# Attention, then a two-layer feed-forward: 16 leftover groups of v summed for four units at once, and the rests of the features moved to GpSimd

## The reference

```python
q_d, k_d, v_d = (t.reshape(B, H, S // 4, 4, D).mean(axis=3) for t in (q, k, v))
out_up = np.repeat(softmax_attention(q_d, k_d, v_d), 4, axis=2)   # pooled: 144 queries, 144 keys
scores = scale * q @ k.T, only where abs(i - j) < 4               # band: 7 keys for each query
out_local = softmax(scores) @ v
x = (out_up + out_local) as (B * S, H * D) = 2304 tokens x 512
h = x @ moe_w_in;  x = (h * sigmoid(h)) @ moe_w_out               # 512 -> 2048 -> 512
h = x @ moe2_w_in; y = (h * sigmoid(1.702 * h)) @ moe2_w_out
```

## Time and profile before

| | |
|---|---|
| median of 3 runs | 808.96 us (808.95 to 809.37) |
| the profiled execution | 808.21 us, span 806.4 us |
| PE busy | 790.0 us (98%) |
| DVE, ACT, POOL busy | 646.0, 530.8, 208.8 us |

### The profile page before, as it was taken

How to read it: one execution, slowest core, us unless ns; L and a number is a source line. 1 busy time by engine, 2 the same in 40 slices (tenths; PEclk the granted TensorE clock), 3 DMA queues, 4 the chain that set the end, 5 groups by cost and what they waited for, 6 DMA issues and landing times.

```text
span 806.4 us, 15771 instructions
## 1 busy us (share of the span) xinstructions
PE 790.0 (98%) x5864; PEld 763.4 (95%) x5864; DVE 646.0 (80%) x905; ACT 530.8 (66%) x849; POOL 208.8 (26%) x203
## 2 busy tenths in 40 slices
PE   9888799999999999999999999999999999999998
PEld 5666599999999999999999999999999999999998
DVE  7999899999898778998678898899555688456466
ACT  5878865677655678555687556678455786465673
POOL 5899977520274220445200000000000000000000
PEclk9999999999999999999999999999999999999999
DMA  8877647787878887677877778868887877878773
GB/s 282 266 249 238 197 150 259 262 298 233 283 236 268 260 315 245 217 261 258 289 267 249 239 250 262 256 224 272 306 275 257 273 249 266 304 250 271 264 256 136
DMA packets 100763, 205.51 MB, mean 255 GB/s; under 512 B 8784, under 2 KB 56400, under 8 KB 100688
## 3 DMA queue, kind: packets, MB, share of 16 engines
q1 hardware_dynamic: 100688, 204.51, 76.0%
HBM read 160.96 MB, written 43.52 MB: 254 GB/s over the span
## 4 chain that ended last, share of the span: by engine, by line
PE 88%; POOL 8%; issue 3%; DVE 1%; ACT 0%; POOLq 0%; DVEq 0%
PE hid L351 43%; PE yp L377 42%; POOL vpair L1038 2%; POOL vavg L1042 1%; PE yp L393 1%; POOL pband L1032 1%; POOL G L1062 1%; POOL G L1063 1%; POOL G L1068 1%; POOL G L1066 1%; POOL x L284 0%; DVE wh L315 0%; PE sc L1342 0%; PE hp L1342 0%; PE pt L1229 0%
## 5 line engine op out<-in xcount | busy, mean ns | idle before, releaser
L351 PE MATMUL hid<-xs,wh 128*128 128x384 f32 x2016 | 351.3, 334 | 0.7 <-issue 0.4
L351 PEld LDWEIGHTS hid<-xs,wh 128*128 128x128 f32 x2016 | 349.3, 188 | 1.7 <-issue 1.4
L377 PE MATMUL yp<-gr,wh 128*128 128x384 f32 x1968 | 342.1, 334 | 0.0
L377 PEld LDWEIGHTS yp<-gr,wh 128*128 128x128 f32 x1968 | 341.2, 188 | 0.1
L306 ACT ACTIVATE wh<-wr 128x1024 fp32r<-128x1024 f32 (+1 forms) x164 | 164.6, 1004 | 149.8 <-PE hid L351 120.0
L569 DVE TENSOR_TENSOR gr<-G,gr 128x768 fp32r<-128x768 f32 x144 | 137.9, 964 | 52.7 <-ACT gr L449 52.7
L449 ACT ACTIVATE gr<-G 128x768 fp32r<-128x768 f32 x144 | 121.8, 845 | 66.9 <-PE yp L377 66.8
L315 DVE TENSOR_TENSOR wh<-wr,wh 128x1024 fp32r<-128x1024 f32 x76 | 95.1, 1251 | 19.0 <-ACT wh L306 18.8
L412 ACT ACTIVATE G<-G 128x1152 f32<-128x1152 f32 x48 | 55.7, 1161 | 0.8 <-DVE G L564 0.8
L533 DVE TENSOR_TENSOR hv<-p,hid 128x384 f32<-128x384 f32 x48 | 26.3, 548 | 29.8 <-PE hid L351 28.0
L559 DVE TENSOR_TENSOR G<-hv,hid 128x384 f32<-128x384 f32 x48 | 26.3, 549 | 28.2 <-PE hid L351 28.2
(11 more groups left out here) (101 smaller groups left out, 748.0 us busy)
## 6 DMA issues: line engine op xcount, KB each, us to landing
wh<-rests SPq DMA_DIRECT2D x72, 512.0 KB, 3.7
wr<-sums_out SPq DMA_DIRECT2D x48, 512.0 KB, 4.7
wr<-in_w_out SPq DMA_DIRECT2D x36, 512.0 KB, 5.2
rests<-wh SPq DMA_DIRECT2D x36, 512.0 KB, 3.5
wr<-sums_in SPq DMA_DIRECT2D x40, 384.0 KB, 4.0
wr<-in_w_in SPq DMA_DIRECT2D x40, 256.0 KB, 3.5
qk<-in_qkT SPq DMA_DIRECT2D x11, 576.0 KB, 4.8
G<-in_w_in SPq DMA_DIRECT2D x12, 512.0 KB, 5.3
```

The lines of the kernel that those rows point to most:

```text
L351: last = eng.matmul(hid[:, at, 0:HALF], lhsT=wh[:, w % SLOTS, part, a % 4, cc * P:(cc + 1) * P], rhs=xs[:, rest, q, cc, :], start=start an ...
L377: last = eng.matmul(yp[:, at + m, 0:HALF], lhsT=wh[:, w % SLOTS, part, p % 4, m * P:(m + 1) * P], rhs=gr[:, p, rest, :], start=start and p ...
```

## The change

The last groups are now 32 instead of 16: a unit's own tile `vn` holds its first 112 groups, in one slot, and the 32 last ones of four units fill one tile of 128 partitions (`vn_last`), which is summed once for four units, into `vlast`. That is done in units 0, 2, 4 and 7, ahead of that unit's own sum. The transposed probabilities and the pooled product are cut at 112 keys instead of at 128, in as many matmuls as before. `vn` needs no zeros, so its two memsets go. The rests of B11, B21, T1, T3 and T2 leave DVE: GpSimd makes those of B11 and B21 whole, in units 5 and 6, and those of T1, T3 and T2 in two halves each, in units 10 to 15. DVE's rests of B22 and T4 at the end now wait for them.

```diff
+        def rest_x(eng, n, q, chunk=None):
             eng.wait_ge(self.x_hi, 7 * n + FILLS.index(q) + 1)
-            eng.tensor_tensor(xs[:, 1, q], features(n, q), xs[:, 0, q].bitcast(F32),
-                              ALU.subtract).then_inc(self.x_lo, 1)
+            at = slice(0, 2) if chunk is None else slice(chunk, chunk + 1)
+            eng.tensor_tensor(xs[:, 1, q, at], features(n, q)[:, at], xs[:, 0, q, at].bitcast(F32),
+                              ALU.subtract).then_inc(self.x_lo if chunk != 0 else self.x_part, 1)
+            if chunk:
+                eng.wait_ge(self.x_part, FILLS.index(q) - 1)
...
-    RESTS = {4: B11, 6: B21, 10: T1, 12: T3, 14: T2}
+    RESTS = {5: (B11, None), 6: (B21, None), 10: (T1, 0), 11: (T1, 1), 12: (T3, 0), 13: (T3, 1), 14: (T2, 0),
+             15: (T2, 1)}
+    LAST_SUMS = {0: 0, 2: 1, 4: 2, 7: 3}
+    LAST_LOADS = {1: 0, 3: 2, 5: 4}
...
+        def summed(n):
+            return n + 1 + sum(i <= n for i in LAST_SUMS)
+        def pooled(u, j):
+            at = u.n % 4 * REST
+            return (slice(0, MOST), slice(0, MOST)) if j == 0 else (slice(MOST, SD), slice(at, at + REST))
...  SyncE
+                    if u.n in LAST_LOADS:
+                        eng.wait_ge(v_sum, summed(LAST_LOADS[u.n]))
+                        load_last(LAST_SUMS[LAST_LOADS[u.n]] + 1)
...  GpSimd, behind pband
+                if u.n in LAST_SUMS:
+                    at = LAST_SUMS[u.n]
+                    eng.wait_ge(last_in, DMA_INC * (at + 1))
+                    sum_groups(vn_last[:], vpair[:], vlast[:, at, :], summed(u.n) - 2)
+                eng.wait_ge(vn_in[u.odd], DMA_INC * (u.half + 1))
                 if u.n > 1:
                     eng.wait_ge(avg_out, u.n - 1)
+                sum_groups(vn[u.odd][0:MOST], vpair[0:MOST], vavg[u.odd][0:MOST], summed(u.n) - 1)
+                if u.n in RESTS:
+                    ffn.rest_x(eng, 0, *RESTS[u.n])
...
+            def sum_groups(groups, pair, to, done):
+                if done:
+                    eng.wait_ge(v_sum, done)
+                eng.tensor_tensor(pair, groups[:, 0:4 * D], groups[:, 4 * D:8 * D], ALU.add).then_inc(v_half, 1)
+                eng.wait_ge(v_half, done + 1)
+                eng.tensor_tensor(to, pair[:, 0:2 * D], pair[:, 2 * D:4 * D], ALU.add).then_inc(v_sum, 1)
...  VectorE
-                elif n in RESTS:
-                    ffn.rest_x(eng, 0, RESTS[n])
                 elif n == UNITS:
                     ffn.rest_weights(eng, 1)
+                    eng.wait_ge(ffn.x_lo, 5)
                     ffn.rest_x(eng, 0, B22)
                     ffn.rest_x(eng, 0, T4)
...
-            for v_rest in vn:
-                eng.memset(v_rest[:, 1, :], 0.0).then_inc(pads, 1)
...  TensorE, avg_product
-                eng.wait_ge(v_sum, u.n + 1)
+                eng.wait_ge(v_sum, summed(u.n))
```

More of the change, by code:

```diff
@@ L100, in __init__ @@
         self.x_half, self.x_sum, self.x_hi, self.x_lo = (sem(n) for n in ("x_half", "x_sum", "x_hi", "x_lo"))
+        self.x_part = sem("x_part")
         self.product, self.pair = sem("product"), sem("pair")
@@ L266, in round_x @@
             eng.activation(xs[:, 0, q], features(n, q), ACT.Copy).then_inc(self.x_hi, 1)
-        def rest_x(eng, n, q):
+        def rest_x(eng, n, q, chunk=None):
             eng.wait_ge(self.x_hi, 7 * n + FILLS.index(q) + 1)
-            eng.tensor_tensor(xs[:, 1, q], features(n, q), xs[:, 0, q].bitcast(F32),
-                              ALU.subtract).then_inc(self.x_lo, 1)
+            at = slice(0, 2) if chunk is None else slice(chunk, chunk + 1)
[3 more added lines that the diff above has]
+                eng.wait_ge(self.x_part, FILLS.index(q) - 1)
         def sum_x(eng, n, q, chunk=None):
@@ L779, in programs, with build @@
         self.round_weights, self.rest_weights = round_weights, rest_weights
-def build(nc, qkT, v, vw, w_in, w_out, out, heads):
+def build(nc, qkT, v, vw, vl, w_in, w_out, out, heads):
     B, H, S, D = heads
@@ L823, in build @@
     SC = 512 - HALF * WIN
-    REST = SD - P
+    REST = P // 4
+    MOST = SD - REST
     NA = 3
@@ L872, in build @@
             VN = FACTOR * 2 * D
[L873 to L877, removed]
+            vlast = sb("vlast", [P, UNITS // 4, 2 * D])
+            vavg = [sb(f"vavg{i}", [P, 2 * D]) for i in range(2)]
+            vn = [sb(f"vn{i}", [P, VN]) for i in range(2)]
+            vn_last = sb("vn_last", [P, VN])
+            vpair = sb("vpair", [P, 2 * D * 2])
             sums4 = sb("sums4", [P, 2, SD])
@@ L914, in build @@
         vn_in = [sem(f"vn_in{i}") for i in range(2)]
+        last_in = sem("last_in")
         qk_in = [sem(f"qk_in{i}") for i in range(3)]
@@ L947, in load_vn, with load_last @@
             def load_vn(u):
[L948 to L952, removed]
+                eng.dma_start(vn[u.odd][0:MOST], v[bass.ds(u.n, 1), :, :].rearrange("a p n -> (a p) n")).then_inc(
+                    vn_in[u.odd], DMA_INC)
+            def load_last(i):
+                eng.dma_start(vn_last[:], vl[bass.ds(i, 1), :, :].rearrange("a p n -> (a p) n")).then_inc(
+                    last_in, DMA_INC)
             def load_vwin(u):
@@ L963, in start @@
                 load_vn(u)
+                load_last(0)
                 load_qk(u.after().after())
@@ L1033, in body @@
                                   ALU.mult).then_inc(b_nrm, 1)
[L1034 to L1039, removed]
+                if u.n in LAST_SUMS:
[3 more added lines that the diff above has]
+                eng.wait_ge(vn_in[u.odd], DMA_INC * (u.half + 1))
                 if u.n > 1:
                     eng.wait_ge(avg_out, u.n - 1)
-                eng.tensor_tensor(vavg[u.odd][:], vpair[:, 0], vpair[:, 1], ALU.add).then_inc(v_sum, 1)
+                sum_groups(vn[u.odd][0:MOST], vpair[0:MOST], vavg[u.odd][0:MOST], summed(u.n) - 1)
+                if u.n in RESTS:
+                    ffn.rest_x(eng, 0, *RESTS[u.n])
                 if not first:
@@ L1068, in sum_weights @@
                     eng.tensor_tensor(at(S4), at(A12), at(S2), ALU.subtract).then_inc(ffn.w0_sum, 1)
-            eng.wait_ge(pads, 5)
+            eng.wait_ge(pads, 3)
             iterations(eng, lambda u: None, body)
@@ L1084, in group @@
                 else:
-                    eng.activation(pta[:, j - NLG, :], src[:, 0:NA * AR], ACT.Copy).then_inc(p_cp, 1)
+                    rows = pooled(u, j - NLG)[1]
+                    eng.activation(pta[rows, j - NLG, :], src[rows, 0:NA * AR], ACT.Copy).then_inc(p_cp, 1)
             def body(u, first, last):
@@ L1100, in body @@
                 if last is None:
-                    eng.wait_ge(v_sum, UNITS)
+                    eng.wait_ge(v_sum, summed(UNITS - 1))
                     ffn.scalar(eng, True)
@@ L1281, in group @@
                 else:
+                    keys, rows = pooled(u, j - NLG)
                     for c in range(NA):
-                        keys = (j - NLG) * REST
-                        last = transpose(to[:, c * AR:(c + 1) * AR], pavg[u.odd][:, c, keys:keys + P])
+                        last = transpose(to[0:rows.stop, c * AR:(c + 1) * AR],
+                                         pavg[u.odd][:, c, keys.start - rows.start:keys.stop])
                 last.then_inc(p_tr, 1)
@@ L1305, in avg_product @@
                 eng.wait_ge(p_cp, 3 + NG * (u.n + 1))
-                eng.wait_ge(v_sum, u.n + 1)
+                eng.wait_ge(v_sum, summed(u.n))
                 for h in range(2):
-                    for j in range(2):
-                        last = eng.matmul(po[h * D:(h + 1) * D, OA:OA + SD], lhsT=vavg[u.odd][:, j, h * D:(h + 1) * D],
-                                          rhs=pta[:, j, :].rearrange("p (c q) -> p c q", c=NA)[:, :, h * QT:h * QT + AQ],
+                    for j, pool in enumerate((vavg[u.odd], vlast[:, u.n // 4, :])):
+                        rows = pooled(u, j)[1]
+                        last = eng.matmul(po[h * D:(h + 1) * D, OA:OA + SD], lhsT=pool[rows, h * D:(h + 1) * D],
+                                          rhs=pta[rows, j, :].rearrange("p (c q) -> p c q", c=NA)[
+                                              :, :, h * QT:h * QT + AQ],
                                           start=(j == 0), stop=(j == 1))
@@ L1381 @@
                              axis=1).reshape(B * H // 2, P, -1)
+    groups = pairs.reshape(B * H // 2, S // 4, 8 * D)
     named = dict(
         qkT=np.stack([q, k]).transpose(1, 2, 4, 0, 3).reshape(B * H // 2, 2 * D, 2, S),
-        v=pairs.reshape(B * H // 2, S // 4, 8 * D), vw=windows,
+        v=groups[:, :112], vw=windows, vl=groups[:, 112:].reshape(-1, P, 8 * D),
         w_in=np.stack([quarters_in(moe_w_in), quarters_in(moe2_w_in)]),
```

## The result

The changed kernel takes 818.89 us (818.4 to 819.23, 4 runs) against 808.98 us: ratio 1.0121, interval 1.0103 to 1.0139, 9.9 us slower. The forecast was 808.4 with a range up to 811.0: wrong in sign and outside the range. The profiled execution has a span of 816.6 us, 10.2 more than before. As in the prediction, P7 is the start of `pband` in unit 7 on GpSimd, and the seam is the stretch from P15 to the feed-forward's long run on PE.

The account below looks back on a forecast made before the run. GpSimd, back to back in attention's second half, delays PE's always-busy stretch. Starting unit 15 3.85 us earlier, with most given back before the feed-forward, gains 0.6 us: span 807.6, so 808.4 us against the runs, range 806.9 to 811.0.

Parts of the forecast that it names:

- P7: Start of pband in unit 7 on GpSimd, forecast at 49.35 us, 0.9 earlier than before.
- the seam: From P15 to the feed-forward on PE: T2's rest, finished in unit 15, holds PE; 9.4 us, feed-forward at 106.06.
- P15: Start of pband in unit 15 on GpSimd, forecast at 96.66 us against 100.51 before: 3.85 us gained.
- an edit costed at nothing: Matmuls of the pooled product cut at 112 keys: same columns, not on the path, so no time gained or lost.
- GpSimd's prices: Steps on GpSimd: 0.81 us for adding 256 values, 0.42 for 128, 0.96 for a half rest in fp32r.
- Rival C: Rests on GpSimd dearer than L284; at twice the price 816.5 us; chance 0.14.
- The walk of the units: Unit starts on GpSimd and DVE: DVE's 5.63 us paces early units, GpSimd's 5.85 units 10 to 14.
- P10: Start of pband in unit 10 on GpSimd, forecast at 67.39 us, with 0.7 us to spare.
- Rival B: PE's clock falls to 1.2 GHz in its 3.2 us idle; 12 matmuls take 2.1 us more: 810.5; chance 0.10.

Follow-up runs that it names:

- e1: The kernel before with one edit: the second product of pooled v reads only partitions 96 to 127 instead of 128; 815.39 us, ratio 1.0081.
- e2: The changed kernel with the last groups' product on all 128 partitions, from four buffers zero outside their 32 rows; 811.94 us, ratio 1.0038.
- e3: The changed kernel with the pooled product's loops exchanged: both heads on 112 rows, then both on 32; 812.58 us, ratio 1.0046.
- e12: The kernel before with the second product of pooled v on partitions 64 to 127; 815.34 us, ratio 1.0082.
- e6: e5 with the last tile of 32-group sums in unit 8 instead of 7; 805.56 us, ratio 0.9961.
- e5: e2 with T2's rest made whole in unit 14 on GpSimd instead of in halves in 14 and 15; 807.46 us, ratio 0.9983.
- e14: The changed kernel with T2's rest made whole in unit 14, the 32-row products still alternating; 817.37 us, ratio 1.0102.
- e7: e2 with nine matmuls of zeros in PE's idle time at the seam; 811.33 us, ratio 1.0038.
- e4: The kernel before with only the rests of B11, B21, T1, T3 and T2 moved to GpSimd, pooled v as before; 817.09 us, ratio 1.0102.

## Why the prediction was wrong

The step that failed is an edit costed at nothing: "The matmuls have the same columns. None of these can gain: none is on the path." Both halves failed. The columns are the same, but the row heights alternate, 0.90 us a product. And the product is on a loop that no sum had looked at. With the kernel before and this edit alone the loop is 6.39 us (e1), so without it 5.49, which is what the kernel before takes from its first pooled product to its second; from then on DVE's 5.63 covers it. The cover was 0.14 us. The change added 0.90 for the product and, in most units, 0.13 for ACT's second copy, which the prediction did not look at either: 6.52. The figure of 5.55 in the expectation of e1 was taken from the chain with the product's end counted in, and lies between the loop of before and that of the changed kernel with the old product (5.62, e2). The prediction named what hides its other edits; for this one it did not, and nothing in its rows gave the loop's length.

The trace of before did show that a change of the tile is not free. PE's weight load for the next scores, behind the pooled product, idles 0.20 us where the tile goes from `128*64` to `128*128`:

```profile
93.24 0.11 PEld L1235 LDWEIGHTS sc<-band,ident 128*128 128x128 bf16 x2 [0.20 <-issue]
```

In this row the tile's columns change and its rows do not; the price of the rows was in no row of before. The rule stood in the Trainium skill ("TensorEngine Tiling (Array Packing)", Tiling Modes, Key Properties: changing the mode, not only the tile, makes TensorE drain), and the forecast did not use it. It gives no price; e1, e3 and e12 agree with it.

Point by point:
- GpSimd's prices were right: 0.42 for 128 values (0.41), 0.96 for half a rest in fp32r. Rival C, that it would be dearer, is refuted.
- The walk of the units was right where PE does not pace: P7 within 0.07, units 10 to 14 at 5.85 (e2). It was 1.1 us short in unit 7: there DVE did not get in between GpSimd's queued sums. The next 1.2 us of e2, up to P10, came with it and went with it in e6 (unit 9: 6.26 and 4.95); their way was not isolated.
- The seam was right: T2's rest holds PE (e5: 4.5 us; e14: 1.5), 9.4 us forecast. At a full clock and on 128 rows it is 9.31 (e7). That the changed kernel's own seam is 9.5 is in part luck: T2's rest was ready 3.4 us behind P15 instead of 4.3, since here VectorE's weight rest came too late to hold GpSimd, and unit 15's product takes 0.9 more.
- Rival B (clock) was not at work in the changed kernel, where PE waited only 0.87 us for T2's rest and the granted clock stayed at 1.00 (110 to 113). It was in e2, e3 and e4. Its price was over-estimated: 1.35, not 2.1.
- The time of rival C, 816.5, lay near the measured one by another cause: it asked for slower rests on GpSimd, and they are not slower.

## What to carry to other kernels

Before calling a matmul's edit free, look at its row height beside its neighbours': keep matmuls on tiles of one height together, or pad a short operand with zeros. Work out each loop through every engine, not only the pace of the busiest; a loop 0.14 us short of the bound is a bound for the first edit that touches it. A rest moved to a less loaded engine must also be ready where the next stage begins: one unit earlier was worth 4.5 us.

## What the runs showed of the hardware

- Matmuls on tiles of 128 or 112 rows alternating with 32, or of 128 with 64: 1.55 us for eight records, 0.65 without; grouped by height 0.79 (e1, e12, e3). 112 and 128 in turn: 0.65 (e2).
- Two ACT copies of 336 values start 0.33 us apart, and 0.46 where the first is of partitions 0 to 111 and the second of 32 that do not begin at partition 0.
- PE idle for 2.7 us after six matmuls: the granted clock next was 0.53, and 12 matmuls took 3.40 us (e2). With 0.76 idle after nine fillers it stayed at 1.00, and they took 2.38 (e7).
- A VectorE subtraction with both inputs in SBUF that came during one of GpSimd's additions took 3.28 us where three were queued (e2), 2.35 where two were (the changed kernel), 1.87 behind one (e6), and 1.21 in the kernel before, where GpSimd's addition, begun 0.15 us earlier, was the one that waited (1.96 instead of 0.73).
